# Local and pooled attention with two gated layers on one core: a second slot of raw input weights, a sum without EPS, and another order around the masks and the transition

## What is computed

```python
def attention(q, k, v):                      # B, H, S, D = 4, 8, 576, 64
    q_d, k_d, v_d = (mean over groups of 4 positions of q, k, v)
    out_up = repeat(sm_attn(q_d, k_d, v_d), 4)
    mask = abs(pos[:, None] - pos[None, :]) < 4
    scores = where(mask, scale * q @ k.T, -1e9)
    scores = scores - max(scores, axis=-1)
    attn = exp(scores)
    attn = attn / (sum(attn, axis=-1) + 1e-09)
    return out_up + attn @ v
x = attention(q, k, v)                       # as 2304 x 512
x = (sigmoid(x @ w_gate) * (x @ w_val)) @ w_out          # 512 -> 1536 -> 512
h = x @ w_in2
out = (h * sigmoid(1.702 * h)) @ w_out2                  # 512 -> 2048 -> 512
```

## Time and profile before

| | us |
|---|---|
| median of three runs (lowest, highest) | 909.59 (908.54, 912.97) |
| the profiled execution, own time | 909.52 |
| its span, first to last instruction | 907.7 |
| TensorE matmuls busy | 892.2 (98%) |
| GpSimd busy | 694.1 (76%) |
| VectorE busy | 517.4 (57%) |
| ScalarE busy | 481.9 (53%) |
| mean granted TensorE clock | 0.996 |

### The profile page before, as it was taken

One profiled execution on the slowest core, in us unless ns is written; L12 is line 12 of the kernel. 1 busy time (PEld: TensorE's weight loads), 2 busy tenths in 40 slices (PEclk: granted clock), 3 DMA queues, 4 the chain that ended last, 5 costly groups with the idle time before them and its releaser, 6 DMA issues.

```text
span 907.7 us, 17629 instructions
## 1 busy us (share of the span) xinstructions
PE 892.2 (98%) x6566; PEld 833.1 (92%) x6566; DVE 517.4 (57%) x975; ACT 481.9 (53%) x964; POOL 694.1 (76%) x547
## 2 busy tenths in 40 slices
PE   8989999999999999999999999999999999999998
PEld 6777789999999999998989999999999898988987
DVE  5767645555555555566565555555665656565565
ACT  5767655454445455455555455554555554544542
POOL 5768689999779999778787679998777877565641
PEclk9999999999999999999999999999999999999999
DMA  9856122222222222211212122422222121232111
GB/s 320 242 176 192 49 70 70 71 70 70 70 71 70 70 71 70 71 70 47 94 47 81 59 70 70 140 71 70 70 70 70 52 88 47 93 117 74 67 47 70
DMA packets 26516, 79.59 MB, mean 88 GB/s; under 512 B 3136, under 2 KB 3136, under 8 KB 26432
## 3 DMA queue, kind: packets, MB, share of 16 engines
q1 hardware_dynamic: 26432, 78.48, 26.3%
HBM read 73.75 MB, written 4.72 MB: 86 GB/s over the span
## 4 chain that ended last, share of the span: by engine, by line
PE 94%; POOL 2%; DVE 2%; issue 1%; ACT 1%; ACTq 0%; POOLq 0%
PE o_ps L402 39%; PE d_ps L414 7%; PE d_ps L412 7%; PE d_ps L415 7%; PE s_ps L412 6%; PE s_ps L414 6%; PE s_ps L415 6%; PE t_ps L414 3%; PE t_ps L415 3%; PE t_ps L412 3%; PE o_ps L375 1%; PE o_ps L395 1%; DVE o_tok L1019 1%; PE d_ps L327 1%; PE t_ps L387 1%
## 5 line engine op out<-in xcount | busy, mean ns | idle before, releaser
L1147 DVE TENSOR_TENSOR att<-o_ps,att 128x512 f32<-128x512 f32 (+1 forms) x246 | 153.0, 625 | 150.6 <-PE o_ps L402 150.6
L1339 POOL TENSOR_TENSOR w_lo<-w_sum,w_hi 128x1024 fp32r<-128x1024 f32 x60 | 144.2, 2404 | 65.0 <-ACT w_hi L708 65.0
L1334 POOL TENSOR_TENSOR w_lo<-w_raw,w_hi 128x768 fp32r<-128x768 f32 x60 | 110.8, 1847 | 29.2 <-ACT w_hi L704 29.2
L414 PE MATMUL d_ps<-xs_lo,w_hi 128*128 128x384 f32 x360 | 120.9, 336 | 0.0
L412 PE MATMUL d_ps<-xs_hi,w_hi 128*128 128x384 f32 x360 | 120.7, 335 | 0.0
L415 PE MATMUL d_ps<-xs_hi,w_lo 128*128 128x384 f32 x360 | 120.7, 335 | 0.0
L1350 POOL TENSOR_TENSOR v_lo<-v_raw,v_hi 128x1024 fp32r<-128x1024 f32 x42 | 100.9, 2403 | 24.5 <-ACT v_hi L712 24.5
L1314 POOL TENSOR_TENSOR w_sum<-w_raw 128x256 f32<-128x256 f32 x120 | 88.5, 738 | 37.0 <-PE t_ps L415 28.7
L402 PE MATMUL o_ps<-v_hi,g_lo 128*128 128x512 f32 x288 | 114.0, 396 | 0.0
L402 PE MATMUL o_ps<-v_lo,g_hi 128*128 128x512 f32 x288 | 113.6, 394 | 0.0
L402 PE MATMUL o_ps<-v_hi,g_hi 128*128 128x512 f32 x288 | 111.9, 389 | 0.0
(11 more groups left out here) (120 smaller groups left out, 2053.8 us busy)
## 6 DMA issues: line engine op xcount, KB each, us to landing
v_raw<-in_w_out_dram SPq DMA_DIRECT2D x42, 512.0 KB, 3.5
w_raw<-in_w_gate_val_dram SPq DMA_DIRECT2D x36, 512.0 KB, 3.4
w_raw<-in_w_in_dram SPq DMA_DIRECT2D x24, 512.0 KB, 3.5
vw<-in_v_win_dram SPq DMA_DIRECT2D x32, 170.6 KB
vt<-in_v_tok_dram SPq DMA_DIRECT2D x16, 320.0 KB, 4.4
qk<-in_q_t_dram SPq DMA_DIRECT2D x16, 288.0 KB, 4.1
qk<-in_k_t_dram SPq DMA_DIRECT2D x16, 288.0 KB, 5.0
out_dram<-att SPq DMA_DIRECT2D x18, 256.0 KB, 4.3
```

Source lines behind the costliest of these rows:

```text
L414: pe.matmul(bank, wh[:, w, cols], xl[:, x, c, :], start=False, stop=False, skip_group_check=True)
L1147: vec.tensor_tensor(part, value, part, ALU.add).then_inc(y_added, 1)
L1334: gp.tensor_tensor(w_lo[b % 2][:, A11:A22 + 1, :], w_raw[:, R11:R22 + 1, :], w_hi[b % 2][:, A11:A22 + 1, :], ALU.subtract).then_inc(wa_rea ...
L1339: gp.tensor_tensor(w_lo[b % 2][:, S1:S4 + 1, :], w_sum[b % 2][:, S1:S4 + 1, :], w_hi[b % 2][:, S1:S4 + 1, :], ALU.subtract).then_inc(ws_re ...
```

## The change

- `w_raw` has two slots; `load_in(b)` waits for block b-2's raw slot only. SyncE issues block 1 at iteration 4 (before: 7), block 2 at 9 and the second output weights, `load_out(1)`, at 10 (before: both after the loop), and all later blocks one block earlier.
- The V windows get one row more per head half, zero but for EPS in the 65th column, and `e` has a column of ones that turns into the matching row of `p_t`. So the product of the values itself gives the sum plus EPS. L1012 and its semaphore go; the reciprocal reads PSUM.
- `p_t` is 64 wide per window, its last 16 columns set to one once, so that weigh writes all 64 partitions; the clearing of `o_ps` goes.
- masks(i+2) stands between weigh(i) and score(i+2); before, masks(i+3) stood at the iteration's end.
- At the transition p6(0) goes ahead of turn_pooled(15) and weigh(15) ahead of p5(0). ScalarE takes snap_p1(0) and the sigmoid's table ahead of drain_pooled(14) and snap_u2(0) behind it, round_in(1) at iteration 8, round_in_sums(1) at 15. VectorE takes c11(0) ahead of add_levels(14). GpSimd takes the four sums of block 1 one by one at iterations 8 to 11, one rest (T3) at 13 instead of 14, and block 2 in the usual order (sums, then rests).

The diff, cut to its core:

```diff
 v_raw = [place(f"v_raw{i}", [P, FG, DM], at=lo_at + 4 * FG * DM * i) for i in range(2)]
-w_raw = place("w_raw", [P, 4, WG])
+w_raw = [place(f"w_raw{i}", [P, 4, WG]) for i in range(2)]
 sig = place("sig", [P, 2, FG, NT])
...
 e = place("e", [P, PAIRS, 2, HK])
-p_t = place("p_t", [P, NWIN, QW])
+p_t = place("p_t", [P, NWIN, HK])
 o_tok = place("o_tok", [P, PAIRS, 2, D])
...
 vt_loaded = sems("vt_loaded", 2)
-w_loaded, v_loaded = sem("w_loaded"), sems("v_loaded", 2)
+w_loaded, v_loaded = sems("w_loaded", 2), sems("v_loaded", 2)
...
         for h in range(2):
-            sp.dma_start(vw[u % 2][HK * h:HK * h + KW].rearrange("p w d -> p (w d)"), v_win[u, KW * h:KW * (h + 1)]
+            sp.dma_start(vw[u % 2][HK * h:HK * h + KW + 1].rearrange("p w d -> p (w d)"), v_win[u, (KW + 1) * h:(KW + 1) * (h + 1)]
                          ).then_inc(vw_loaded[u % 2], 16)
...
-        if b == len(BLOCKS):
+        if b >= len(BLOCKS):
             return
-        if b >= 1:
-            sp.wait_ge(wa_ready, b)
-            sp.wait_ge(wsum_ready, b)
+        if b >= 2:
+            sp.wait_ge(wa_ready, b - 1)
+            sp.wait_ge(wsum_ready, b - 1)
         k, m = BLOCKS[b]
         q, lay, p, g = GROUPS[k]
-        sp.dma_start(w_raw[:, :, :].rearrange("p a n -> p (a n)"), w_gate_val[g, m] if lay == 1 else w_in2[g]
-                     ).then_inc(w_loaded, 16)
+        sp.dma_start(w_raw[b % 2][:, :, :].rearrange("p a n -> p (a n)"), w_gate_val[g, m] if lay == 1 else w_in2[g]
+                     ).then_inc(w_loaded[b % 2], 16)
...
             load_out(0)
-        if i == 7:
+        if i == 4:
             load_in(1)
-    load_in(2)
-    load_out(1)
+        if i == 9:
+            load_in(2)
+        if i == 10:
+            load_out(1)
     load_in(3)
+    load_in(4)
     for k in range(NG):
...
         if k + 1 < NG and layer(k + 1) == 1:
-            load_in(LAST[k + 1] + 1)
+            load_in(LAST[k + 1] + 2)
         if k + 2 < NG:
-            load_in(FIRST[k + 2] + 1)
+            load_in(FIRST[k + 2] + 2)
         for q in (2, 4):
...
                 for h in range(2):
-                    rows = slice(HK * h, HK * h + KW)
-                    mm = pe.matmul(o_ps[HK * par:HK * par + QW, h, pair * VC:(pair + 1) * VC],
+                    rows = slice(HK * h, HK * h + KW + 1)
+                    mm = pe.matmul(o_ps[HK * par:HK * (par + 1), h, pair * VC:(pair + 1) * VC],
                                    p_t[rows, w, :], vw[u % 2][rows, w, :], start=True, stop=True)
...
     score_pooled(1)
-    masks(2)
     turn_pooled(0)
...
         weigh(i)
+        masks(i + 2)
         score(i + 2)
...
         turn_pooled(i + 1)
-        if i + 3 < UNITS:
-            masks(i + 3)
     weigh(last - 1)
...
     weigh_pooled(last - 1)
+    p6(0)
     turn_pooled(last)
-    p6(0)
+    weigh(last)
     pe.wait_ge(exped_d, UNITS)
...
     p5(0)
-    weigh(last)
     p7(0)
...
         for b, pairs in enumerate((range(PT0), range(PT0, PAIRS))):
-            c = nc.scalar.copy(p_t[:, 2 * pairs.start:2 * pairs.stop, :],
+            c = nc.scalar.copy(p_t[:, 2 * pairs.start:2 * pairs.stop, 0:QW],
                                t_ps[:, b, 0:len(pairs) * P].rearrange("p (w k) -> p w k", k=HK)[:, :, 0:QW])
...
-        act.wait_ge(w_loaded, 16 * b + 16)
+        act.wait_ge(w_loaded[b % 2], 16 * (b // 2) + 16)
         if b >= 2:
             act.wait_ge(in_done[b % 2], NP * (b // 2))
-        nc.scalar.copy(w_hi[b % 2][:, A11:A22 + 1, :], w_raw[:, R11:R22 + 1, :]).then_inc(wahi_ready, 1)
+        nc.scalar.copy(w_hi[b % 2][:, A11:A22 + 1, :], w_raw[b % 2][:, R11:R22 + 1, :]).then_inc(wahi_ready, 1)
...
             round_out(0)
+        if i == 8:
+            round_in(1)
         if i == 9:
...
             round_x_sum(0, T4, 3)
+        if i == last - 1:
+            snap_p1(0)
+            nc.scalar.activation(token[:, 1:2], token[:, 0:1], ACT.Sigmoid)
         if i == last:
-            round_in(1)
-            snap_u2(0)
-            nc.scalar.activation(token[:, 1:2], token[:, 0:1], ACT.Sigmoid)
+            round_in_sums(1)
             sig11(0)
...
         if i == last - 1:
-            snap_p1(0)
+            snap_u2(0)
         if i + 2 < UNITS:
...
             copy_values(i + 2)
-    round_in_sums(1)
     sig22(0)
...
         dve.wait_ge(weighed, u + 1)
-        vec.tensor_scalar(den[:, :].rearrange("p (h a) -> p h a", h=2), sums[:, :, :, D], EPS, 0.5, ALU.add, ALU.max
-                          ).then_inc(den_ready, 1)
-        dve.wait_ge(den_ready, u + 1)
-        vec.reciprocal(inv[:, :], den[:, :]).then_inc(inv_ready, 1)
+        vec.reciprocal(inv[:, :].rearrange("p (h a) -> p h a", h=2), sums[:, :, :, D]).then_inc(inv_ready, 1)
         dve.wait_ge(inv_ready, u + 1)
...
         vec.memset(qk[slot][:, 1, PAD + S:S + 2 * PAD], 0.0)
-    vec.memset(e[:, :, :, KW:HK], 0.0)
+    vec.memset(e[:, :, :, KW:KW + 1], 1.0)
+    vec.memset(e[:, :, :, KW + 1:HK], 0.0)
     vec.memset(d_ps[:, 1, VS_AT:VS_AT + P], 0.0)
     vec.memset(t_ps[:, 1, (PAIRS - PT0) * P:2 * SD], 0.0)
-    vec.memset(o_ps[:, :, :], 0.0).then_inc(zeroed, 1)
+    vec.memset(p_t[:, :, QW:HK], 1.0).then_inc(zeroed, 1)
     dve.wait_ge(edges_ready, 1)
...
     inverse_pooled(UNITS - 1)
+    c11(0)
     add_levels(UNITS - 2)
-    c11(0)
     normalise(UNITS - 1)
...
-        x = gp.tensor_tensor(w_sum[b % 2][:, name, :], a, c, op)
-        return x
-
-    def sums_in_begin(b):
-        raw, into = w_raw, w_sum[b % 2]
-        pool.wait_ge(w_loaded, 16 * b + 16)
+        return gp.tensor_tensor(w_sum[b % 2][:, name, :], a, c, op)
+
+    def sum_in_1(b):
+        pool.wait_ge(w_loaded[b % 2], 16 * (b // 2) + 16)
         if b >= 2:
             pool.wait_ge(in_done[b % 2], NP * (b // 2))
-        sum_in(b, S1, raw[:, R21, :], raw[:, R22, :], ALU.add).then_inc(wsum_step, 1)
+        sum_in(b, S1, w_raw[b % 2][:, R21, :], w_raw[b % 2][:, R22, :], ALU.add).then_inc(wsum_step, 1)
+
+    def sum_in_2(b):
         pool.wait_ge(wsum_step, 2 * b + 1)
-        sum_in(b, S2, into[:, S1, :], raw[:, R11, :], ALU.subtract).then_inc(wsum_step, 1)
-
-    def sums_in_end(b):
-        raw, into = w_raw, w_sum[b % 2]
-        sum_in(b, S3, raw[:, R11, :], raw[:, R21, :], ALU.subtract)
+        sum_in(b, S2, w_sum[b % 2][:, S1, :], w_raw[b % 2][:, R11, :], ALU.subtract).then_inc(wsum_step, 1)
+
+    def sum_in_3(b):
+        sum_in(b, S3, w_raw[b % 2][:, R11, :], w_raw[b % 2][:, R21, :], ALU.subtract)
+
+    def sum_in_4(b):
         pool.wait_ge(wsum_step, 2 * b + 2)
-        sum_in(b, S4, raw[:, R12, :], into[:, S2, :], ALU.subtract).then_inc(wsum_ready, 1)
+        sum_in(b, S4, w_raw[b % 2][:, R12, :], w_sum[b % 2][:, S2, :], ALU.subtract).then_inc(wsum_ready, 1)
...
         pool.wait_ge(wahi_ready, b + 1)
-        gp.tensor_tensor(w_lo[b % 2][:, A11:A22 + 1, :], w_raw[:, R11:R22 + 1, :], w_hi[b % 2][:, A11:A22 + 1, :],
+        gp.tensor_tensor(w_lo[b % 2][:, A11:A22 + 1, :], w_raw[b % 2][:, R11:R22 + 1, :], w_hi[b % 2][:, A11:A22 + 1, :],
                          ALU.subtract).then_inc(wa_ready, 1)
...
     def split_in(b):
-        sums_in_begin(b)
-        sums_in_end(b)
+        sum_in_1(b)
+        sum_in_2(b)
+        sum_in_3(b)
+        sum_in_4(b)
         low_in(b)
...
         if i == 2:
-            sums_in_begin(0)
+            sum_in_1(0)
+            sum_in_2(0)
         if i == 3:
-            sums_in_end(0)
+            sum_in_3(0)
+            sum_in_4(0)
         if i == 4:
...
             sum_t1(0)
-            sums_in_begin(1)
+            sum_in_1(1)
         if i == 9:
...
             sum_t2(0)
+            sum_in_2(1)
         if i == 10:
             sum_t4(0)
+            sum_in_3(1)
         if i == 11:
             sum_t3(0)
+            sum_in_4(1)
         if i == 12:
...
             low_x_sum(0, T1, 5)
+            low_x_sum(0, T3, 6)
         if i == 14:
-            low_x_sum(0, T3, 6)
             low_x_sum(0, T4, 7)
     low_x(0, B22, quarter[1, 1], 3)
-    sums_in_end(1)
     low_in(1)
     low_in_sums(1)
-    low_in(2)
-    sums_in_begin(2)
-    sums_in_end(2)
-    low_in_sums(2)
+    split_in(2)
     low_out(0)
...
     v_pad[:, :, :, D] = 1.0
-    ins["v_win"] = pack(_np.stack([v_pad[:, :, QW * w:QW * w + KW] for w in range(NWIN)], 3).reshape(UNITS, 2 * KW, NWIN * VC))
+    v_end = _np.zeros((UNITS, 2, 1, VC), v.dtype)
+    v_end[:, :, :, D] = EPS
+    v_win = [_np.concatenate([v_pad[:, :, QW * w:QW * w + KW], v_end], 2) for w in range(NWIN)]
+    ins["v_win"] = pack(_np.stack(v_win, 3).reshape(UNITS, 2 * (KW + 1), NWIN * VC))
     v_t = _np.zeros((UNITS, VT * P, P), v.dtype)
...
```

More of the change, by code:

```diff
@@ L135, in attention_mlp_kernel @@
         warm = place("warm", [P, 2 * P], BF16)
-        small = place("small", [P, 6 * PAIRS + 26])
-        nmax, den, inv = (small[:, 2 * PAIRS * i:2 * PAIRS * (i + 1)] for i in range(3))
-        nmax_d, bias_d, den_d0, den_d1, plus_d, inv_d = (small[:, 6 * PAIRS + 4 * i:6 * PAIRS + 4 * (i + 1)] for i in range(6))
```

(7 more changed lines are left out.)

## The result

The change makes the kernel slower: 934.25 us (933.45 to 934.41, five runs) against 911.11 for the kernel before in the same runs, ratio 1.0258 (95% interval 1.0239 to 1.0277). The forecast was 904.7, its range ended at 908.5, and no rival lay higher than 917.8.

What follows compares the result with a forecast made beforehand. TensorE was taken to work gaplessly from about 135 us, leaving only attention, held by the copy, and the transition to gain. Terms -0.9 - 0.6 + 0.5 - 0.4 - 2.0 + 0.3 - 1.7 = -4.8 gave 904.7, range 901.5 to 908.5.

Steps and rivals of the forecast that it cites:

- Widths: Attention: 64-column weight loads, the wider-pitched copy and one more V window row cost 0; load bound +13 us.
- (e): Rival: 64-column weight loads of the values aren't hidden in any attention unit, +13 us, 917.8; chance 0.03.
- Masks after the values: Attention units: moving the masks gains 0.10 us a unit, limited by the copy; nine units, -0.9 us.
- Masks and pauses: Attention: values start 0.28 us earlier, masks passing within pauses without a semaphore; two pauses at -0.3, -0.6 us.
- The copy holds the pooled product: Attention units: the pooled product waits for ScalarE's copy of the turned weights, 1.73 us behind the turn.
- Rival (c): The copy doesn't hold the attention unit; 12 units gain 0.37 us each, -4.4, 901.8; chance 0.04.
- Normalising: Attention, VectorE: L1012 goes, some 0.21 us, the reciprocal reads PSUM; counted 0 for itself.
- Loads moved: Attention: SyncE's earlier weight loads meet instruction transfers before two pauses; +0.5 us, between 0 and +2.
- Rival (d): Loads at iterations 4 and 10 lengthen two attention pauses and the clock falls: +3.2 us, 907.9; chance 0.08.
- Transition: Attention's end to block 2: p6 first -0.4 us, block 2's wait gone -2.0, L1350 +0.3, no clock fall -1.7.
- Rival (b): The wait at the transition moves instead of going, the clock falls again: -1.4 us, 908.1; chance 0.20.
- Rival (a): Attention's first half-clock stretch goes too, the pause at 46.6 shortening from 2.2 to 1.9: -1.7 us, 903.0; chance 0.20.

Runs made afterwards that it cites:

- e1: The kernel before with only its V window transfers changed, 57 rows per head half instead of 56, the added row zero and unread: 935.3 us, ratio 1.0276.
- e6: The kernel after with 56-row V window transfers and the values' stationary operand 48 columns wide again: 906.03 us, ratio 0.9964.
- e2: The kernel after with V window transfers of 56 rows again, the EPS row loaded once into each slot: 907.1 us, ratio 0.9966.
- e7: The kernel after with 56-row V window transfers, masks back at the iteration's end and 48 columns for the values: 905.35 us, ratio 0.9957.
- e5: The kernel after with 56-row V window transfers and masks back at the iteration's end: 906.28 us, ratio 0.9961.
- e9: e2 with sum_values(i+2) put ahead of weigh_pooled(i) in TensorE's list: 915.56 us, ratio 1.006.
- e10: e7 with sum_values(i+2) put ahead of weigh_pooled(i) in TensorE's list: 911.91 us, ratio 1.0017.
- e11: e7 with VectorE's addition and maximum (L1012) back in front of the reciprocal, which reads SBUF again: 906.11 us, ratio 0.9954.
- e8: The kernel after with 56-row V window transfers and SyncE's loads in their old order, two slots kept: 908.71 us, ratio 0.9991.
- e3: The kernel after with V windows of 64 rows per head half, the seven added rows zero and unread: 912.77 us, ratio 1.0029.
- e4: The kernel before with V windows of 63 rows per head half, the seven added rows zero and unread: 917.4 us, ratio 1.008.

## Why the prediction was wrong

**The step that failed** stands in *Widths*: "The V windows have one row more on 56: 0". Only the bytes, 2% more, speak for the 0, and it had no bounds. The row number sets how many engines carry the transfer; 57 puts it on 3. Measured: 27.0 us on the kernel before by the start of the 15th pooled turn (e1), of the 28.6 that the whole change lost there. No rival had it: the only slower one, (e), put its +8 on the weight loads, which cost 0.03 a unit (e6) instead of its 0.8. The row needed was on the page of before: 200 transfers on 16 engines would bring 3200 small packets and there were 3136, so some already ran on fewer, and that was a reason to ask what 57 would do.

**With that step right** the change is e2_after_56_rows, 907.1, inside the range and 2.4 over the forecast. The rest, by its own terms:
- *Masks after the values*: wrong by 0.28 a unit. "the turn (L348) starts at the same distance from L360 as before, 2.36, for the same work stands between": it is 2.64, as the masks cost 0.51 between values and scores and 0.29 in front of the values, and the 64 columns 0.03. The unit was forecast at 6.02 and takes 6.30; 6.02 is what it takes with masks left where they were and 48 columns (e7). Nine units of 0.28 would be 2.5, about the 2.4 missing, but that fit is luck: e5 takes 0.25 a unit back and is only 0.8 faster.
- *Masks and pauses*, -0.6: the way was right, the size wasn't. The pauses without a semaphore take 5.4 us in the kernel before and 3.5 in e2, 1.9 less. With the masks back at the iteration's end they take 7.5 (e5) and 5.3 (e7), which eats up much of what the shorter unit gives.
- *The copy holds the pooled product*, 1.73 behind the turn: right (e2, e5). Rival (c) needed this wait gone; e9 and e10 took it away and lost time all the same.
- *Normalising*: 0.10 a unit, right (e7, e11), and without an effect on the time that can be told. The forecast took a gain in the unit's rhythm for a gain in time; in e5 and e10 longer pauses took such gains back.
- *Loads moved*, +0.5: no cost shown; back in the old order the time was 1.6 higher (e8). Rival (d), longer pauses by the loads, is refuted by the same sums of pauses.
- *Transition*: -0.4 - 2.0 + 0.3 - 1.7 = -3.8 forecast, 802.2 - 798.4 = 3.8 measured, and by its terms too. From the 15th pooled turn to the last product ahead of block 2 it took 0.47 less, the wait and its hand-over gave 2.15, the clock 1.4 more, and 0.3 came back later. Rival (b) is refuted, if barely: GpSimd's L1341 ran from 155.05 to 157.45 in the kernel after, and TensorE started block 2 at 157.51 without a wait.
- *Rival (a)*, the first half-clock stretch goes as well: in the profiles it did once the rows were 56 (e2, e5 to e8, e11). The pause in front of it was 2.2 with a fall, 1.93 in e11 without one, 1.94 in e3 and e4, 2.88 and 3.67 with one. One pause of 2.44 in e9 had none, so its length alone doesn't tell. The stretches also differ between executions of one kernel: the mean clock was 1.000 in all executions of e2 and e6, but 0.996 to 1.000 in e5. And 36 of the 53 executions of the kernel before that ran beside the experiments had 0.997 or 0.998, which is one stretch, where its profile has two.

## What to carry to other kernels

Before the outer size of a transfer is changed, by a single row even, factor it: the largest divisor up to 16 is the number of engines that carry it, and the fullest engine's bytes per round, at the rate that a busy stretch shows, must stay under the compute's round. That isn't enough where several rounds are loaded at once: 63 rows were under it and still cost 0.8%. A constant row can be loaded once and kept out of the repeated transfer. And where pauses without a semaphore stand in a stage, don't count a shorter round as time won: measure it, as the fastest list here (5.92) was slower than the one at 6.12.

The best version tried is e7: the change with 56 rows per transfer, masks where they were and 48 columns, 905.35 us, ratio 0.9957 (0.9942 to 0.9972); e2, e5, e6 and e11 can't be told from it.

## What the runs showed of the hardware that was not expected

- A transfer of 57 rows ran on 3 engines, 56 on 14, 63 on 9, 64 on 16, and the 3 held up transfers behind them that use all 16: V in token order landed 11.6 us after its issue instead of 4.4.
- Two matmuls of masks cost 0.22 us more between the values and the scores than in front of the values. Rows show where (0.87 to the masks, 0.39 to the scores, against 0.75 without them), not why.
- TensorE ran out of instructions after the same records, for up to 3.7 us. The pauses without a semaphore take 3.5 us in all with a unit of 6.30 (e2) and 8.7 with one of 5.92 (e10); but e3, at 6.30, has 7.4, so the unit's length alone doesn't set them.
